# A new order for the first batch of a three-stage mixer, with its scan pattern in PSUM and its head pairs' loads on 120 partitions

## What is computed

```python
# attention, per batch and head, t = 0..767
state = alpha[t][:, None] * state + outer(k[t], v[t])      # 48 x 48
y[t] = q[t] @ state
# second stage, x = y as (batch, 768, 384); U 768x32, V 32x768
u = x + ((x^T @ U) @ V)^T
x2 = u + relu(u @ w_ch1) @ w_ch2                            # 384 -> 1536 -> 384
# third stage
theta = x2 @ w_theta
u = x2 + tok_r @ (x2 * cos(theta)) + tok_i @ (x2 * sin(theta))
out = u + relu(u @ w_ch)
```

## Time and profile before

| | us |
|---|---|
| median of 3 runs | 667.65 (667.53 to 671.77) |
| profiled execution, its own time | 669.96 |
| its span | 668.1 |
| TensorE busy in the span | 651.9 (98%) |
| VectorE | 331.8 (50%) |
| ScalarE | 259.5 (39%) |
| GpSimd | 252.5 (38%) |

### The profile page before, as it was taken

The page is one execution under the profiler, slowest core; times in us unless marked ns, Lnnn a source line. Parts: engine busy times, 40 slices in busy tenths (PEclk is TensorE's granted clock), DMA queues, the critical chain, the costliest instruction groups (busy, mean ns, idle before and its releaser), DMA issues.

```text
span 668.1 us, 15759 instructions
## 1 busy us (share of the span) xinstructions
PE 651.9 (98%) x6360; PEld 624.4 (93%) x6360; DVE 331.8 (50%) x540; ACT 259.5 (39%) x540; POOL 252.5 (38%) x253
## 2 busy tenths in 40 slices
PE   7899999999999999999999999999999999999998
PEld 4568899999999999999999999999999999999998
DVE  8947875237654236564232125665435543554522
ACT  5655544323444333444233344344324421432320
POOL 5776662113332113332111572246323631633220
PEclk9999999999999999999999999999999999999999
DMA  9535403006203006200013531130032014002101
GB/s 334 188 140 211 171 2 127 2 1 214 91 3 127 1 1 233 71 30 11 1 36 100 186 129 48 36 119 25 0 112 93 8 42 146 24 0 82 60 1 71
DMA packets 24873, 54.73 MB, mean 82 GB/s; under 512 B 2160, under 2 KB 16752, under 8 KB 24816
## 3 DMA queue, kind: packets, MB, share of 16 engines
q1 hardware_dynamic: 24816, 53.90, 23.3%
HBM read 44.45 MB, written 9.44 MB: 81 GB/s over the span
## 4 chain that ended last, share of the span: by engine, by line
PE 89%; DVE 5%; issue 3%; ACT 2%; POOL 1%; DMA 0%; DVEq 0%; ACTq 0%; POOLq 0%
PE banks L753 23%; PE banks L1140 21%; PE banks L783 21%; PE banks L1212 6%; PE banks L1058 5%; PE banks L396 3%; PE banks L1115 2%; PE banks L522 2%; PE banks L514 2%; PE banks L457 2%; DVE state L485 1%; PE banks L701 1%; PE banks L647 1%; DVE tail L345 1%; DVE tokiL L248 1%
## 5 line engine op out<-in xcount | busy, mean ns | idle before, releaser
L767 DVE SCALAR_TENSOR_TENSOR hidL<-banks,hidH 128x384 fp32r<-128x384 f32 x96 | 53.4, 556 | 119.1 <-ACT hidH L763 119.0
L753 PE MATMUL banks<-uH,w1H 128*128 128x384 f32 x288 | 100.0, 347 | 0.4 <-ACT uH L733 0.4
L783 PE MATMUL banks<-hidH,w2H 128*128 128x384 f32 x288 | 96.8, 336 | 2.1 <-ACT x_nat L634 0.7
L753 PE MATMUL banks<-uL,w1H 128*128 128x384 f32 x288 | 96.6, 335 | 0.0
L783 PE MATMUL banks<-hidH,w2L 128*128 128x384 f32 x288 | 96.5, 335 | 0.0
L753 PE MATMUL banks<-uH,w1L 128*128 128x384 f32 x288 | 96.4, 335 | 0.0
L783 PE MATMUL banks<-hidL,w2H 128*128 128x384 f32 x288 | 96.2, 334 | 0.0
L763 ACT ACTIVATE hidH<-banks 128x384 fp32r<-128x384 f32 x96 | 47.0, 490 | 90.0 <-PE banks L753 90.0
L1198 POOL TENSOR_TENSOR u2L<-x_res,u2H 128x384 fp32r<-128x384 f32 x24 | 24.5, 1020 | 95.4 <-ACT u2H L1192 95.4
L382 POOL TENSOR_TENSOR k_end<-qka_sb,tail 112x384 f32<-112x384 f32 x32 | 30.0, 938 | 75.2 <-DVE tail L345 74.2
L783 PEld LDWEIGHTS banks<-hidH,w2H 128*128 128x128 f32 x288 | 54.1, 188 | 4.2 <-issue 3.3
(11 more groups left out here) (130 smaller groups left out, 1414.5 us busy)
## 6 DMA issues: line engine op xcount, KB each, us to landing
qka_sb<-qka SPq DMA_DIRECT2D x30, 579.5 KB, 5.5
v_sb<-v_nat SPq DMA_DIRECT2D x32, 144.0 KB, 5.3
stage<-w SPq DMA_DIRECT2D x6, 768.0 KB, 4.5
x_dram<-u_t SPq DMA_DIRECT2D x8, 576.0 KB, 3.8
x_f<-x_dram SPq DMA_DIRECT2D x12, 384.0 KB, 4.4
x_res<-x_dram SPq DMA_DIRECT2D x8, 576.0 KB, 4.3
out_t<-stage SPq DMA_DIRECT2D x24, 192.0 KB, 1.9
stage<-tok_r_t SPq DMA_DIRECT2D x3, 768.0 KB, 4.7
```

The source lines that it names most:

```text
L753: last = nc.tensor.matmul(ps[:, 0:HALF], w[:, f, P * k:P * (k + 1)], x[half][:, k, :], start=(k == 0 and i == 0), stop=(k == DM_TILES - 1 ...
L767: nc.vector.scalar_tensor_tensor(hidL[s % 2][:], hid_ps[s % 2][:, 0:HALF], 0.0, hidH[s % 2][:].bitcast(F32), ALU.max, ALU.subtract).then_i ...
L783: last = nc.tensor.matmul(acc[m][:, 0:HALF], w[:, f, P * m:P * (m + 1)], x[s % 2][:], start=(f == 0 and i == 0), stop=(f == F_TILES - 1 an ...
```

## The change

It rewrites the order of batch 0 on every engine and changes the layout of alpha:

- A slot becomes 66 elements: a zero, 64 alphas, a zero. `restart` and `rel_start` become one tile `pattern` (bank 6 in batch 0): ones at the last element of a slot start the backward scan, reciprocals at the first element start the forward scan. So in batch 0 both scans read their second input from PSUM, and the reciprocals are written there.
- Loads of `qka` take 120 rows instead of 128. Rows 112 to 119 are still read by nobody.
- VectorE: mask of u+1 before `state` of u.
- TensorE: updates of u+1 before carried of u; one `keep_warm` call instead of two, for units 0 to 2 only; from unit 3 on G in pieces of one head pair and one token half (96 columns, three matmuls), pairs 0 to 2 in bank 7, pair 3 in bank 1; a new order of the low-rank turns and products after the last unit.
- ScalarE: U and V in four parts (units 3 to 6), weight parts from unit 2 on, a new order at the end.
- GpSimd follows the new tables of weight parts.
- SyncE: the first weights before unit 4, U and V after it; unit 7 after weights 1.

```diff
-SLOT = SUB + 1
+SLOT = SUB + 2
+LOADED = 120
...
-                sp.dma_start(qka_sb[i][:], qka[b, u, :, 0:ROW]).then_inc(S[f"qka_in{i}"], 16)
+                sp.dma_start(qka_sb[i][0:LOADED, :], qka[b, u, 0:LOADED, 0:ROW]).then_inc(S[f"qka_in{i}"], 16)
...
+        def pattern_of(b):
+            return bank[6] if first_batch(b) else pattern
...
-            nc.vector.reciprocal(rel_start[0:PAIR_ROWS, 0:SCAN:SLOT], tail[u % 2][0:PAIR_ROWS, :, 0]
+            nc.vector.reciprocal(pattern_of(b)[0:PAIR_ROWS, 0:SCAN:SLOT], tail[u % 2][0:PAIR_ROWS, :, 0]
...
-            nc.vector.tensor_tensor_scan(flat(rel[0:PAIR_ROWS]), alpha_of(u)[:, 0:SCAN], rel_start[0:PAIR_ROWS, :], 0.0,
+            nc.vector.tensor_tensor_scan(flat(rel[0:PAIR_ROWS]), alpha_of(u)[:, 0:SCAN], pattern_of(b)[0:PAIR_ROWS, 0:SCAN], 0.0,
...
+        EARLY_G = 3 * PAIR_DIM
+
+        def g_bank(pair):
+            return bank[7] if PAIR_DIM * pair < EARLY_G else bank[1]
+
+        def first_g(pe, u):
+            pe.wait_ge(S["y_done"], u + 1)
+            pair, half = divmod(u, 2)
+            cols = slice(PAIR_DIM * pair, PAIR_DIM * (pair + 1))
+            for c in range(CPH):
+                last = nc.tensor.matmul(g_bank(pair)[0:3 * RANK, cols], u_three[half][:, c, :], x_nat[:, CPH * half + c, cols],
...
-        EARLY_AT = (range(0, 0), range(0, 0), range(0, 0), range(0, 0), range(0, 1), range(1, 2), range(2, 4), range(4, 6))
-        AHEAD_HI = (range(6, 8), range(8, 10))
-        SLOT_HI = {s: (2 * s + 10, 2 * s + 11) for s in range(7)}
-        AHEAD_LO, FIRST_LO = range(6, 8), range(8, 10)
+        EARLY_AT = (range(0, 0), range(0, 0), range(0, 1), range(1, 2), range(2, 3), range(3, 4), range(4, 6), range(6, 7))
+        AHEAD_HI = (range(7, 10), range(10, 13))
+        SLOT_HI = {s: (2 * s + 13, 2 * s + 14) for s in range(5)} | {5: (23,)}
+        AHEAD_LO, FIRST_LO = range(7, 10), range(10, 13)
...
-        SMALL_AT = (3, 4)
+        SMALL_AT = (3, 4, 5, 6)
...
-        KEEP_WARM = 2
+        KEEP_WARM = 1
+        FIRST_G_AT = 3
...
+            load_weight(sp, 0)
+            load_unit(sp, 0, 4)
+            load_v(sp, 0, 4)
+            for a in range(2):
+                sp.dma_start(u_raw[a], u_w[:, a, :]).then_inc(S["u_loaded"], 16)
+            sp.dma_start(v_raw, v_w).then_inc(S["v_loaded"], 16)
+            load_unit(sp, 0, 5)
+            load_v(sp, 0, 5)
+            sp.wait_ge(S["tail_done"], 5)
+            load_unit(sp, 0, 6)
+            load_v(sp, 0, 6)
+            sp.wait_ge(S["rel_done"], 5)
             load_weight(sp, 1)
+            sp.wait_ge(S["rel_done"], 6)
+            load_unit(sp, 0, 7)
+            load_v(sp, 0, 7)
+            sp.wait_ge(S["tail_done"], 7)
             load_weight(sp, 2)
...
             for u in range(UNITS):
                 act_updates(act, 0, u)
+                if u == UNITS - 1:
+                    first_g_hi(act, bank[7], slice(0, EARLY_G), "early_g_ready", "early_g_hi_done")
                 if u:
                     act_output(act, 0, u - 1)
...
+            act_output(act, 0, UNITS - 1)
             act_lr_hi(act, 0, 0, 0)
+            first_g_hi(act, g_bank(PAIRS - 1), slice(EARLY_G, MODEL), "g_ready", "g_hi_done")
+            act_lr_x(act, 0, 0, 2)
             act_lr_hi(act, 0, 0, 1)
...
-                dve_state(dve, 0, u)
                 if u + 1 < UNITS:
                     dve_mask(dve, 0, u + 1)
+                dve_state(dve, 0, u)
...
+                    for w in range(0 if u == FIRST_G_AT else u - 2, u - 1):
+                        first_g(pe, w)
                 pe_values(pe, 0, u).then_inc(S["half_done"], 1)
+                pe_state(pe, 0, u + 1)
+                if u == UNITS - 2:
+                    first_g(pe, UNITS - 3).then_inc(S["early_g_ready"], 1)
                 pe_carried(pe, 0, u).then_inc(S["y_ready"], 1)
-                pe_state(pe, 0, u + 1)
+            pe.wait_ge(S["rel_done"], UNITS)
+            lr_turn(pe, 0, 0, 0).then_inc(S["first_turned"], 1)
+            pe.wait_ge(S["updates_done"], updates_before(0, UNITS - 1))
+            pe.wait_ge(S["mask_done"], UNITS - 1)
+            lr_turn(pe, 0, 0, 1).then_inc(S["first_turned"], 1)
+            pe_values(pe, 0, UNITS - 1).then_inc(S["half_done"], 1)
+            pe.wait_ge(S["x_t_done"], 1)
+            lr_turn(pe, 0, 0, 2).then_inc(S["first_turned"], 1)
+            pe.wait_ge(S["x_t_done"], 2)
+            first_g(pe, UNITS - 2)
+            pe_carried(pe, 0, UNITS - 1).then_inc(S["y_ready"], 1)
```

More of the change, by code:

```diff
@@ L101, in mixer_kernel @@
         state = [sa(f"state{i}", [P, HEAD_DIM, PLACES]) for i in range(2)]
-        restart = sa("restart", [P, SCAN + 1])
+        pattern = sa("pattern", [P, SCAN + 1])
         causal = sa("causal", [P, SUB])
@@ L372, in queries @@
             wait(eng, S["y_ready"], q_free(b, u))
-            ops.tensor_tensor(q_slot(u)[0:PAIR_ROWS, :, HEAD_DIM:], q_of(u), rel[0:PAIR_ROWS, :, 1:SLOT], ALU.mult
+            ops.tensor_tensor(q_slot(u)[0:PAIR_ROWS, :, HEAD_DIM:], q_of(u), rel[0:PAIR_ROWS, :, 1:SUB + 1], ALU.mult
                               ).then_inc(S["q_rel_done"], 1)
@@ L381, in pool_keys @@
             wait(pool, S["scores_ready"], n - 1)
[L382 removed]
+            nc.gpsimd.tensor_tensor(subs_of(k_end[s][0:PAIR_ROWS, :]), k_of(u), tail[s][0:PAIR_ROWS, :, 1:SUB + 1],
                                     ALU.mult).then_inc(S["k_end_done"], 1)
@@ L641, in pe_g @@
             g_products(pe, range(TOK_TILES)).then_inc(S["g_ready"], 1)
[L643 to L648, removed]
+        EARLY_G = 3 * PAIR_DIM
[7 more added lines that the diff above has]
+                last = nc.tensor.matmul(g_bank(pair)[0:3 * RANK, cols], u_three[half][:, c, :], x_nat[:, CPH * half + c, cols],
+                                        start=(half == 0 and c == 0), stop=(half == 1 and c == CPH - 1),
+                                        skip_group_check=True)
             return last
@@ L681, in lr_banks @@
             if first_batch(b) and half == 0:
-                return ((bank[6], bank[7]), (bank[0], bank[1]), (bank[6], bank[7]))[m]
+                return ((bank[6], bank[0]), (bank[1], bank[2]), (bank[6], bank[7]))[m]
             return bank[0], bank[1]
@@ L1371, in _ @@
                                     pattern=[[1, SUB]], channel_multiplier=-1).then_inc(S["setup_pool"], 1)
-            nc.gpsimd.memset(restart[:], 0.0).then_inc(S["setup_pool"], 1)
+            nc.gpsimd.memset(pattern[:], 0.0).then_inc(S["setup_pool"], 1)
             for i in range(2):
@@ L1375, in _ @@
             pool.wait_ge(S["setup_pool"], 6)
-            nc.gpsimd.memset(restart[:, 0:SCAN + 1:SLOT], 1.0).then_inc(S["setup_pool"], 1)
+            nc.gpsimd.memset(pattern[:, SLOT - 1:SCAN:SLOT], 1.0).then_inc(S["setup_pool"], 1)
             for i in range(2):
@@ L1427, in _ @@
                     act_k_nat(act, 0, u + 1)
-                if u == UNITS - 2:
-                    first_g_hi(act, bank[7], slice(0, EARLY_G), "early_g_ready", "early_g_hi_done")
+                if u == UNITS - 1:
                     act_lr_x(act, 0, 0, 0)
@@ L1599 @@
     slots = qka[..., 2 * HALF:2 * HALF + SCAN].reshape(BATCH, UNITS, P, SUBS, SLOT)
-    slots[..., 1:] = rows[..., 2 * HALF:].reshape(BATCH, UNITS, P, SUBS, SUB)
+    slots[..., 1:SUB + 1] = rows[..., 2 * HALF:].reshape(BATCH, UNITS, P, SUBS, SUB)
     qka[..., 2 * HALF:2 * HALF + SCAN] = slots.reshape(BATCH, UNITS, P, SCAN)
```

78 lines of the change are left out of this document (22 added, 56 removed).

## The result

| | before | after |
|---|---|---|
| median, us | 667.78 (667.53 to 671.77) | 678.01 (675.95 to 678.26) |
| ratio | 1 | 1.0135 (95%: 1.0098 to 1.0171) |
| profiled execution, us | 669.96 | 678.26 |
| its span, us | 668.1 | 676.3 |
| landmark (last k = 2 product of slot 0) | 50.92 | 59.52 |

The change made the kernel 10.2 us slower by the medians and 9.0 us by the ratio; 663.4 us was forecast. The landmark says at once where to look: it is 8.6 us late, and all that follows it takes as long as before (668.1 - 50.92 = 617.2 us, 676.3 - 59.52 = 616.8 us). So the loss lies ahead of the landmark, in batch 0's attention and the low-rank product behind it.

What follows compares the result with a forecast made beforehand. VectorE's queue was taken to bound batch 0 until about 31 us, TensorE from 50.92 us on. Gains of 1.3 us (scans) and 2.9 us (end of batch 0) sum to 4.2, giving 663.4 us, range 661.9 to 665.0.

Steps and rivals of the forecast that it cites:

- Bounds: nothing, or one sixteenth of 5.6 us, 0.35 us; I take nothing: Batch 0's loads: cutting 128 rows to 120 was taken to gain nothing, at most 0.35 us.
- Rival D: Loads: 120 rows do nothing measurable; their opposite, fifteen engines, delays unit 2 by 0.4 us; part of the forecast, no separate chance.
- the queue of transfers is full: Start of batch 0: given, with v and weights still using 128 rows, as reason to expect no gain from shorter loads.
- Later loads have room: Loads after unit 2: unit 7's was to land at 26.9 us, with `tail` wanting it at 28.8.
- plus 0.48: Batch 0's scans: `state`, issued behind a running GpSimd product, waits 0.48 us longer, making the period 3.91 us.
- Rival A: Batch 0: the wait does not move to `state`; period 3.43 us, or 3.59 where ScalarE leads; 661.3 us, chance 0.17.
- last product E+13.55: End of batch 0: landmark 13.55 us after E, the end of state(5), against 16.45 before, saving 2.9 us.
- rival B: End of batch 0: the chain from state(5) stays as long, only 1.3 us are gained; 666.3 us, chance 0.18.
- Each part that is wrongly ordered costs at most one instruction of 0.5 to 1.0 us: End of batch 0: the ground for bounding its saving between 1.5 and 4 us.
- rival C: Start: fewer warm-up products drop TensorE's clock to 1.2 GHz, costing 9.5 us in full; 673.0 us, chance 0.05.
- about 1.4: Profile sign in batch 0: `state` takes about 1.4 us; 0.93 would speak for the rival without a moved wait.
- TensorE's clock 1.00 in all stretches: Profile sign: TensorE's granted clock was expected at 1.00 throughout the changed kernel.

Runs made afterwards that it cites:

- experiment 1: The changed kernel with its q, k, alpha loads put back from 120 to 128 rows: 673.16 us, 1.0046 times the kernel before.
- experiment 4: The changed kernel with 128-row loads and, on VectorE in batch 0, `state` ahead of the mask again: 665.41 us, 0.9936 times the kernel before.
- experiment 12: The changed kernel with 128-row loads and `state` ahead of the mask, run once more in another series: 665.61 us, 0.9963 times the kernel before.
- experiment 2: The kernel before with only its q, k, alpha loads cut from 128 to 120 rows: 674.07 us, 1.0063 times the kernel before.
- experiment 3: The changed kernel with loads of 112 rows instead of 120: 673.87 us, 1.007 times the kernel before.
- Experiment 5: The kernel before with each q, k, alpha load split into two transfers of 64 rows: 677.14 us, 1.0115 times the kernel before.
- experiment 6: The kernel before with only the new 66-element slot and the pattern in PSUM, its own order and 128 rows: 668.95 us, 0.9999 times the kernel before.
- experiment 10: The changed kernel with 128 rows, `state` before mask, a reordered end, and unit 7's load ahead of weights 1: 668.5 us, 0.9986 times the kernel before.

## Why the prediction was wrong

The landmark was forecast at 46.65 and came at 59.52 us, 12.9 late. Three terms make that up: 5.2 + 4.1 + 3.6 us.

**The loads, 5.2 us: the step "Bounds: nothing, or one sixteenth of 5.6 us, 0.35 us; I take nothing".** State(5) ends at 42.36 us with 120 rows and at 37.16 with 128 (experiment 1). The prediction priced the rows by bytes and by the rows that an engine carries, and took it for certain that a row costs the same in either form. Rival D, "fifteen engines that delay unit 2 by one fifteenth", made the same assumption: 0.4 us was its price for one load. A packet of one whole row took 0.310 instead of 0.206 us, and unit 2's load landed after 8.0 us in place of 5.6. No row of before showed a transfer of other than 128 rows beside one of 128, so both bounds lacked a ground; a form that the trace doesn't show should have been bounded by what a full queue loses at a lower rate. The prediction itself said "the queue of transfers is full"; there every per cent of a packet counts for each of the loads behind it. That "Later loads have room" was read with the rates of before: `tail` waited 1.23 and 1.70 us for the loads of units 4 and 5.

**The wait of `state`, 4.1 us: the step "plus 0.48", with its period of 3.91 us.** Forecast for state(5) 33.1, with whole loads 37.16. The mechanism was right, and for units 0 and 1 so was the size (1.47 and 1.45 us, period 3.95). What was left out stood in the change itself: the new table puts weight parts from unit 2 on, on GpSimd right behind the query product, and `state` then takes up to 2.42 us. The step put `state` behind "a running GpSimd product" and didn't ask what GpSimd issues next. Three periods of 4.9 instead of 3.91 carry 3.0 of the 4.1 us; the last one, 4.95 where 4.30 was forecast, and a start 0.4 us late carry the rest. The Trainium skill ("SBUF — State Buffer", section "Who interferes with whom") has the two engines exclude each other for an instruction, the first to start winning. The forecast weighed that rule as one instruction's wait, and the runs show two in a row: 1.46 us behind one, 2.42 behind two.

The same rule pointed to the way out. Rival A asked for a period of 3.43 us and got a chance of 0.17 as something that might happen by itself. It takes one moved line: `state` issued 0.16 us ahead of the query product (experiment 4).

**The end, 3.6 us: the step "last product E+13.55".** Measured from the end of state(5), it was E+17.16 in the changed kernel and E+17.0 in experiment 1; even with the better order (experiment 4) E+16.36, against 16.45 before. So rival B, "The end does not pay", was right about this part. By the steps, in experiment 4: state(6) was early (E+3.2 against 3.9); state(7) ended at E+7.3, not 5.8 to 6.2, and took 2.01 us, 1.1 of it held by GpSimd's low part of V; carried(7) ended at E+9.4, not 7.9; uL(0) began at E+11.0, not 9.25; the landmark came 5.4 us behind that, not 4.3. In that last stretch VectorE's uL(2) took 1.23 us against GpSimd's weight part, and its u_t had waited 2.50 us for the third product. Each of these steps slipped by an instruction or two, and the bound "Each part that is wrongly ordered costs at most one instruction of 0.5 to 1.0 us" was applied to the whole chain once. The 0.6 to 0.8 us between experiment 4 and the kernels with E+17.0 and E+17.16 go with a `state` still behind the mask and a lower clock; no run parts the two.

**Right:** `rel` at 0.98 us; the mask immune behind GpSimd; a first `state` of 1.46 against "about 1.4"; nothing to gain or lose behind the landmark; rival C not decisive up to 30 us. Wrong was "TensorE's clock 1.00 in all stretches": it was 0.83 from 10 to 30 us and 0.50 from 45 to 50. From 10 to 15 us it was still 1.00 while TensorE worked for only 2.65 of 5 us, and 0.66 in the next 5. With the same single warm-up call experiments 4 and 12 had 0.91 and 1.00 from 10 to 30 us and 1.00 from 30 to 50.

That 4.2 us were forecast as a gain and 4.3 are there in experiment 4, another kernel, is luck. The route is another too: state(0) ends 0.8 us earlier, the five periods give 3.3, and the end 0.1 where 2.9 were forecast. Three sums of the prediction are off by at most 0.1 us, which changes nothing: 11.45 + 0.9 + 1.1 is 13.45 and not 13.55, the port is free at 2.98 and not 2.96 us, and rival C's 9.5 us give 672.9 and not 673.0.

**What was only inferred.** That the form of a transfer sets its rate is shown (experiments 1, 2, 3 and 5). Why is not: the traces don't say which engine wrote which rows. The Trainium skill ("SBUF — State Buffer", section "Can I just issue two DMAs to hit both halves?") says that the ports are picked by a single transfer's span of rows, that two transfers side by side brought only 6% over one, and that all sixteen ports take one transfer over all 128 rows. Experiment 5 agrees (232 and 238 GB/s in two halves from 5 to 15 us, 386 and 404 whole), and it is the rule that the prediction should have set beside the count of engines. By the map of ports on the same page of the Trainium skill (section "Door 1: The DMA port swizzle") rows 0 to 119 reach all sixteen ports, worked out from its table, so by the map alone the 120 rows should be fast, and the measurement (249 to 261 GB/s from 5 to 15 us) decides against that reading. The Trainium skill ("DMA: Bandwidth & Descriptors", section "The descriptor swizzle") says that in a 128-row transfer each engine writes one port. If with 120 rows each engine took eight neighbouring rows, engines would meet at shared ports. That would fit the rates of 120 rows, but it stays an inference.

## What to carry to other kernels

Leave a load at all 128 partitions even where some rows are read by nobody: cutting 6% of the bytes cost 4 to 9 us here, and where the queue of transfers is full, a transfer's form is worth more than its size. Then look at the first instruction that waits for a load: only there does a slower rate cost time (experiment 3 against 1). Where VectorE and GpSimd exclude each other, follow both queues to the next two instructions, and issue VectorE's two-input SBUF instruction ahead of GpSimd's, not behind: GpSimd can pay off the path. And shortening an instruction on the fullest engine can gain nothing while the engines that feed it keep their order (experiment 6: 0; with the new order 4.3 us, of which no run shows the order's own share).

## What the runs showed of the hardware

- The time of a packet of one whole row (4636 or 4660 bytes), from 5 to 20 us with the queue full or nearly so: 0.183 us in the kernel before and 0.206 in experiment 1 with 128 rows, 0.310 with 120 rows, 0.276 with 112, 0.308 in two halves of 64. Between 10 and 15 us the queue moved 404 GB/s with 128 rows (experiment 1) and 261 with 120 (the change). A lone load: 579.5 KB in 3.6 us, 582.5 in 3.8, 546.1 in 4.7 (120 rows), 509.7 in 4.4 (112 rows).
- GpSimd products that follow one another at once keep a VectorE scan with two SBUF inputs out through both: 0.93 us alone, 1.46 behind one, 2.40 to 2.42 behind two. If the scan starts first it takes 0.93 us, and GpSimd's product 1.50.
- The mask and the PSUM-fed scans ran at 0.53 to 0.56 and 0.94 to 0.98 us inside GpSimd's products in batch 0 of every kernel here.
- TensorE stood idle for 3.4 us inside one group of products without a releaser (experiment 10), not explained.
